# Reordering SyncE's queue around attention heads 2 to 5, with the first MLP's early weights loaded behind later heads

## The reference, cut to what matters

```python
# attention: 2 batches x 8 heads, 768 tokens, head size 64, 16 centroids per head
q_assign = argmax(q_n @ c_n.T); k_assign = argmax(k_n @ c_n.T)
scores = where(q_assign == k_assign, q @ k.T / 8, -1e9)
attn = softmax(scores) @ v                       # 16 heads in all
# first MLP: x [1536, 512], w_in [512, 2048], w_out [2048, 512]
h = x @ w_in; g = (a0 + a1 h + a2 h^2 + a3 h^3) / (1 + |b0||h| + |b1| h^2); x = g @ w_out
# second MLP: w_gate, w_val [512, 1536], w_out [1536, 512]
out = (silu(x @ w_gate) * (x @ w_val)) @ w_out
```

## Time and profile before

| | |
|---|---|
| median of 3 runs | 790.48 us (790.32 to 793.43) |
| profiled execution | 791.54 us, of which the profile's span is 789.8 us |
| PE busy | 781.8 us, 99% of the span |
| DVE, ACT, POOL busy | 570.1, 516.6, 523.5 us |
| TensorE clock granted | full speed in every slice |

### The profile page before, as it was taken

One profiled execution on the slowest core, in us unless ns is written; L12 is line 12 of the kernel. 1 busy time (PEld: TensorE's weight loads), 2 busy tenths in 40 slices (PEclk: granted clock), 3 DMA queues, 4 the chain that ended last, 5 costly groups with the idle time before them and its releaser, 6 DMA issues.

```text
span 789.8 us, 12696 instructions
## 1 busy us (share of the span) xinstructions
PE 781.8 (99%) x4241; PEld 701.3 (89%) x4241; DVE 570.1 (72%) x1047; ACT 516.6 (65%) x957; POOL 523.5 (66%) x457
## 2 busy tenths in 40 slices
PE   9999999999999999999999999999999999999998
PEld 8889999999998888888888888899999999999997
DVE  6989999999996788777777877655545545554453
ACT  5878888888887787776777889644544434333322
POOL 4777998898585899222222288888889876665620
PEclk9999999999999999999999999999999999999999
DMA  9786555463311700000000011242111114211102
GB/s 210 170 221 149 143 152 131 107 156 103 88 58 35 224 9 1 1 0 1 1 0 1 1 54 54 67 147 55 27 54 54 41 40 134 54 28 53 27 1 81
DMA packets 57681, 57.92 MB, mean 73 GB/s; under 512 B 6608, under 2 KB 44304, under 8 KB 57616
## 3 DMA queue, kind: packets, MB, share of 16 engines
q1 hardware_dynamic: 57376, 56.52, 26.8%
q10 hardware_dynamic: 240, 0.59, 0.3%
HBM read 33.59 MB, written 3.15 MB: 47 GB/s over the span
## 4 chain that ended last, share of the span: by engine, by line
PE 93%; DVE 3%; issue 1%; POOL 1%; DMA 1%; SPq 0%; ACT 0%; POOLq 0%
PE ps L1156 19%; PE ps L1158 19%; PE ps L1157 18%; PE ps L1310 7%; PE ps L1252 4%; PE ps L1253 4%; PE ps L1325 4%; PE ps L1251 4%; PE ps L1327 4%; PE ps L1289 4%; PE ps L1292 3%; PE ps L1379 2%; DVE neg_max L1081 1%; PE ps L1152 1%; DMA qk_raw<-in_k 1%
## 5 line engine op out<-in xcount | busy, mean ns | idle before, releaser
L544 POOL TENSOR_TENSOR den<-den,mag 128x512 f32<-128x512 f32 x48 | 62.4, 1300 | 121.4 <-ACT den L723 121.2
L1158 PE MATMUL ps<-x_hi,w_lo 128*128 128x512 f32 (+1 forms) x384 | 139.4, 363 | 0.0
L1156 PE MATMUL ps<-x_hi,w_hi 128*128 128x512 f32 (+1 forms) x384 | 139.3, 363 | 0.0
L603 POOL TENSOR_TENSOR w_lo<-w_raw,w_hi 128x768 fp32r<-128x768 f32 (+1 forms) x48 | 101.8, 2129 | 56.4 <-ACT w_hi L776 56.4
L1157 PE MATMUL ps<-x_lo,w_hi 128*128 128x512 f32 (+1 forms) x384 | 139.1, 362 | 0.0
L622 POOL TENSOR_SCALAR prob<-prob,row_inv 128x768 f32<-128x768 f32 x96 | 86.0, 913 | 32.9 <-DVE row_inv L1098 32.4
L863 ACT ACTIVATE probT_hi<-ps 128x384 fp32r<-128x384 f32 x192 | 84.2, 490 | 31.2 <-PE ps L1310 30.0
L1106 DVE TENSOR_TENSOR probT_lo<-ps,probT_hi 128x384 fp32r<-128x384 f32 x192 | 96.8, 546 | 5.9 <-ACT probT_hi L863 5.5
L1081 DVE TENSOR_REDUCE neg_max<-ps 128x1 f32<-128x768 f32 x96 | 91.2, 951 | 8.4 <-PE ps L1292 8.2
L845 ACT ACTIVATE prob<-ps,neg_max 128x768 f32<-128x768 f32 x96 | 86.9, 905 | 3.5 <-DVE neg_max L1081 2.3
L1310 PE MATMUL ps<-ident,prob 128*128 128x128 f32 x576 | 81.5, 276 | 1.2 <-POOL prob L622 1.2
(11 more groups left out here) (147 smaller groups left out, 1991.7 us busy)
## 6 DMA issues: line engine op xcount, KB each, us to landing
k_hihi<-qk_hi SPq DMA_DIRECT2D x32, 192.0 KB, 3.7
w_raw<-in_moe_w_gate SPq DMA_DIRECT2D x48, 128.0 KB, 2.3
w_raw<-in_moe_w_val SPq DMA_DIRECT2D x48, 128.0 KB, 2.6
w_raw<-in_moe_w_in SPq DMA_DIRECT2D x16, 256.0 KB, 3.8
w_raw<-in_moe_w_out SPq DMA_DIRECT2D x16, 256.0 KB, 5.1
qk_raw<-in_q SPq DMA_DIRECT2D x16, 192.0 KB, 3.2
q_hilo<-qk_hi SPq DMA_DIRECT2D x16, 192.0 KB, 3.1
qk_low<-qk_hi SPq DMA_DIRECT2D x16, 192.0 KB, 4.3
```

What stands on the lines that cost most here:

```text
L603: did(g.tensor_tensor(lo[:, wave, :], raw[:, wave, :], hi[:, wave, :].bitcast(F32), ALU.subtract), s_w2lo)
L1156: mm(dst, hi, m_hi, start=start, stop=False)
L1158: return mm(dst, lo, m_hi, start=False, stop=stop)
```

## The change

SyncE's written order around heads 2 to 5 is altered. `load_qk(4)` stands before `copy_hi(2)` and not behind `copy_lo(2)`. `load_qk(5)` stands between `copy_hi(3)` and `copy_lo(3)`, and not at the head of the loop (behind both parameter loads and `load_v(2)`). `load_v(2)` goes before the two parameter loads. In the loop, `load_w1(u)` follows `load_v(u + 5)` and not `load_v(u + 3)`. On POOL, head 4's low part is taken from its split at step 6 and put at step 9, behind the three normalisations that stand there (tiles 6 to 8 by the kernel's step list).

```diff
-    FIRST_V, LOW_3 = -4, 5
+    FIRST_V, FIRST_W1, LOW_AT = -4, 5, {3: 5, 4: 9}
...
             send_cluster(1)
+            load_qk(4)
             copy_hi(2, hi_copies(2))
             copy_lo(2)
-            load_qk(4)
             send_cluster(2)
             load_v(1)
             copy_hi(3, hi_copies(3))
+            load_qk(5)
             copy_lo(3)
+            load_v(2)
             sp.dma_start(a_raw, a[None, :].to_broadcast([P, 4])).then_inc(s_par_in, 16)
             sp.dma_start(b_raw, b[None, :].to_broadcast([P, 2])).then_inc(s_par_in, 16)
-            load_v(2)
             for h in range(3, NH + 1):
...
-                if h + 2 < NH:
+                if 5 < h + 2 < NH:
                     load_qk(h + 2)
                 if h < NH:
                     load_v(h)
-                if h < 3 + EARLY:
-                    load_w1(h - 3)
+                if FIRST_W1 <= h < FIRST_W1 + EARLY:
+                    load_w1(h - FIRST_W1)
...
-                    if h != 3:
+                    if h not in LOW_AT:
                         split_low(h)
-                if step == LOW_3:
-                    split_low(3)
+                for h, when in LOW_AT.items():
+                    if step == when:
+                        split_low(h)
```

## The result

The changed kernel takes 788.88 us (median of 15 runs, 788.61 to 789.88). The kernel before, run 15 times in all, has a median of 791.17 us (790.08 to 795.33). The medians differ by 2.3 us. The ratio of the runs is 0.9966, with a 95% interval of 0.9956 to 0.9976: 0.34% less. The ratio of the medians is 0.9971; the kernel before has some long runs, which its mean counts and its median does not, and the means differ by 2.7 us. The forecast was 788.1 us and a gain of 2.4. The profiled execution went from 791.54 to 789.01 us (789.1 was forecast), its span from 789.8 to 787.3 us (787.4).

What follows compares the result with a forecast made beforehand. PE, busy for 781.8 of 789.8 us, was taken to bound the kernel. Hole 1 (-1.18) and hole 2 (-1.25) sum to -2.4 us, taking the median of 790.48 to 788.1 us, range 786.7 to 790.6.

Steps and rivals of the forecast that it cites:

- Rival B: Nothing arrives at the end: DVE holds an earlier PE at the next tiles, filling hole 1; 790.5 us, chance 0.08.
- hole 2: PE's wait from 52.17 to 53.42 us before head 3's first tile, for its late cluster rows; forecast -1.25 us.
- Parts 1 and 2: Head 4's load earlier (SyncE) and low part later (POOL): either alone should close hole 1, -1.18 us; together they overlap.
- hole 1: PE's wait at tile 6's turn for POOL's first normalisation of step 9, behind head 4's split; forecast -1.18 us.
- Part 3: First weights from head 5 on: 2.31 us leave SyncE's queue before head 3's cluster rows, closing hole 2, -1.25 us.
- Part 4: Earlier `load_qk(5)` on SyncE: worth nothing, as head 5's split on POOL was never late for PE; only cover.
- Part 5: Weights loaded with heads 5 to 8: no cost, 0.6 us to spare at head 8; upper bound 0.75 us overrun.
- rival C: Moved weights hold SyncE's queue in heads 7 and 8, each losing about 2.5 us: 793.1 us, chance 0.06.
- Rival A: Head 3's cluster rows stay late, say behind head 4's six copies; only hole 1 goes: 789.3 us, chance 0.12.

Runs made afterwards that it cites:

- run 15: Not a label but a count: the unchanged kernel before was run 15 times in all, median 791.17 us (790.08 to 795.33).
- first two experiments: The kernel before with head 4's load before head 2's copies (ratio 1.0028) and, separately, with head 4's low part at step 9 (ratio 1.0024).
- third experiment: The kernel before with only the first weights moved, to heads 5 to 8: ratio 0.9978, span 788.3 us.
- fifth experiment: The kernel before with head 4's low part at step 9 and weights with heads 5 to 8, no load moved: median 789.45 us, ratio 0.9962.
- first four experiments: The kernel before with only head 4's load, its low part, or the weights moved; the changed kernel without the weights' move: ratios 1.0028, 1.0024, 0.9978, 0.9969.
- second experiment: The kernel before with only head 4's low part moved to step 9: median 793.60 us, ratio 1.0024.

## Why the prediction was right, point by point

**Bound and places of the holes: right.** All that moved the time lay in the two holes read off the chain and the waits, and neither DVE nor anything behind the attention took the gain back. Rival B is out: head 2 took 14.54 us, and head 8 kept 2.53 of the 2.54 us. The prediction had 14.67 us for head 2 without its hole. In the profiles it takes 14.53, so hole 2 was worth 1.39 us and not 1.25.

**Parts 1 and 2, hole 1 for 1.18 us: right.** 1.16 was measured at head 2's first tile, 1.13 counted from the tile before. That either part alone closes it was shown twice, by doing one alone (first two experiments) and by undoing one (low part at step 6; head 4's load late).

**Part 3, the weights and hole 2: right that it closes, partly by luck in the size.** The prediction took the whole stretch of 2.31 us off SyncE's queue, and in it an issue that was held for 1.73 us. Alone, the weights' part brought the rows only 1.4 us forward (third experiment), because a hold came elsewhere, for 1.42 us in one issue of head 5's load. That was enough, since the landing took 1.9 us there. In the full change the start came 2.25 us earlier, close to 2.31, though the two copies of head 4's k were held in turn (2.10 us, 1.25 before). The rest came with `load_qk(5)`, which the prediction had put at nothing: with the weights moved, the rows began at 43.7 to 44.9 in the five profiles where that load was early, and at 44.9 to 45.1 in the three where it was late, 0.7 us apart in the mean. So two errors cancelled. The landing of 3.2 us lay between the bounds of 2.0 and 3.6, on the slow side of the middle that was taken, and by the same program's 1.8 to 3.2 us it could have been anywhere there. What is shown as the cause of hole 2 is the landing of the last row. With hole 1 closed as well, the weights' part alone leaves 0.8 us of it (fifth experiment); the weights with the load of head 5 end it, and so does putting the rows in front of the copies. What sets the few us from issue to landing is open.

**Part 4, `load_qk(5)` at nothing: wrong, by 0.7 to 1.0 us in the median together with `load_v(2)`.** I costed it only for POOL, which has no wait there, and not for the queue in front of head 3's rows. It closes no further hole in a good run. That it keeps hole 2 closed in the others is likely, but not shown: none of them was profiled, and head 8 had no room either.

**Part 5, the weights' burst with 0.6 us to spare: right that it costs nothing.** PE did not wait at heads 7 and 8. In the changed kernel's profile the last row of head 8 was issued at 119.9 and landed at 122.5, 1.2 us before PE; in one other profile with the same weights (`load_qk(5)` late) it landed at 123.7 and PE was held for 0.2 us. The margin is real and scatters: one more weight there cost 4.1 us in the median and 6.0 us in the profiled run. That is rival C with its mechanism shown, though not in this change; its price was set by the clock as well as by the overrun.

**Rival A was wrongly priced.** If the rows had stayed at their old distance, hole 1's 1.18 us would not have been a gain, as the rows' landing does not move with PE. Its time was 790.5 us and not 789.3. The first two experiments show it: closing hole 1 alone gave nothing, and worse. The drain of head 4's copies, its mechanism, is not what made the rows late: with the copies still in front and only the weights gone they landed in 1.9 us (third experiment), and in 2.9 in the fifth, against 3.6.

**Gain right, level 0.8 us off.** The gain is 2.5 us between the two profiles and 2.3 between the medians, against 2.4. The median itself, 788.88 us, is 0.8 above the forecast of 788.1. That forecast began from the median of 3 runs, 790.48, where 15 runs have 791.17, and took it to lie 1.06 us below the profiled execution; in the changed kernel the two are 0.13 us apart. The ratio shows more gain than the medians because the kernel before scatters upwards. In the 31 runs that went with the first four experiments its spans reach from 788.3 to 795.4 us, those of the changed kernel in 15 runs from 786.8 to 788.1. Of those 31, each with a span above 792.5 had a granted clock of 0.998 or lower. In the profile of the second experiment a hole of 2.2 us at head 3 was followed by the lower clock. That the same happens in the longer runs of the kernel before is likely but not shown, since none of them was profiled. The prediction did not have this part of the gain.

## What to carry to other kernels

Two waits on one engine in a row are not a sum when the second one's release doesn't depend on that engine: the first one's gain only makes the second longer, so close the last one first, or both together. A small transfer that others wait for is late by its issue and by its landing, and the issue alone does not price it: here 16 KB took 1.8 to 3.2 us to land in the same program, and 5.6 us behind 512 KB more, with the issue hardly moved. So leave it a margin of some us and do not count on the middle of a range. And where a queue's order is full of slack but for one group, moving that group forward (the rows ahead of the copies) does as much as moving everything else out of its way. When a part is costed at nothing, look at every queue that it passes through, not only at the engine that uses it.

## What the runs showed of the hardware that was not expected

The clock could fall after a short hole. A PE hole of 2.23 us and one of 2.60 us were each followed by the lower level (0.50 of full speed) with PE already busy again, for 3 and 7 us; a hole of 2.70 us in another profile was not. The two holes of 1.2 us of the kernel before, and those of 1.1 and 0.6 us in the experiments, were not followed by it in the profiles. The fall cost 1.5 us at head 3, less than its hole, and some 3.2 us behind head 8, more than its hole. In the long hole of 5.09 us the level had fallen before PE was back.

The time from issue to landing of a 16 KB cluster row scatters. The last row of head 3 took 1.8 us in two profiles and 3.2 us in a third, of the same program up to there; in the one with 3.2 us the DMA engines were busy for only 0.32 and 0.19 of the microseconds from 47 to 49, around and behind its issue at 47.35. Behind two weights and six copies (some 2.2 MB) the last row of head 8 took 5.6 us, with the engines busy for most of it, though SyncE was hardly held in issuing it.
